# Feed-forward of a routed mixture kernel: second matrix two pieces behind the first, values parted at odd steps, search passes on new steps

## What is computed

```python
scores = scale * np.matmul(q, k.transpose(0, 1, 3, 2)) - np.log(S)
x = np.matmul(1.0 / (1.0 + np.exp(-scores)), v)        # tokens x 768
order = np.argsort(-(x @ w_gate).flatten())            # 8 experts, 224 tokens each
# walk down order: a token goes to the first expert that still has room
h = np.maximum(x[mask] @ w1[e], 0.0)                   # 768 -> 1024
x[mask] = h @ w2[e]                                    # 1024 -> 768
h = x @ w_in                                           # 768 -> 2048
g = np.maximum(h, 0.0) + alpha * np.minimum(h, 0.0)
out = g @ w_out                                        # 2048 -> 768
```

## Time and profile before

| | |
|---|---|
| median of 3 runs | 1059.88 us (1057.77 to 1060.93) |
| the profiled execution | 1057.56 us |
| its span, first to last instruction | 1055.9 us |
| TensorE busy (matmuls) | 971.5 us, 92% |
| VectorE busy | 568.7 us, 54% |
| ScalarE busy | 393.4 us, 37% |
| POOL busy | 187.3 us, 18% |
| mean granted clock | 0.97 of full |

### The profile page before, as it was taken

How to read it: one execution, slowest core, us unless ns; L and a number is a source line. 1 busy time by engine, 2 the same in 40 slices (tenths; PEclk the granted TensorE clock), 3 DMA queues, 4 the chain that set the end, 5 groups by cost and what they waited for, 6 DMA issues and landing times.

```text
span 1055.9 us, 16340 instructions
## 1 busy us (share of the span) xinstructions
PE 971.5 (92%) x6340; PEld 837.9 (79%) x6340; DVE 568.7 (54%) x1289; ACT 393.4 (37%) x629; POOL 187.3 (18%) x202
## 2 busy tenths in 40 slices
PE   4999999806979999899999999999999999999994
PEld 3555555406969898799989998998999999999993
DVE  3344443597566827956953685596448546211110
ACT  3767766501042223355322214542121355222212
POOL 0010011105160010244301014350101326000001
PEclk9999999956989999999999999999999999999998
DMA  9899998407289685956877855579695446966501
GB/s 199 222 265 269 270 265 250 156 17 254 72 236 371 205 225 179 296 133 211 291 283 234 245 169 131 199 233 347 233 243 190 151 123 197 380 231 214 179 1 52
DMA packets 121474, 222.30 MB, mean 211 GB/s; under 512 B 51424, under 2 KB 69216, under 8 KB 121408
## 3 DMA queue, kind: packets, MB, share of 16 engines
q1 hardware_dynamic: 88064, 120.34, 36.7%
q0 software_dynamic: 21280, 91.59, 28.1%
q10 hardware_dynamic: 12064, 9.47, 3.6%
HBM read 184.84 MB, written 36.52 MB: 210 GB/s over the span
## 4 chain that ended last, share of the span: by engine, by line
PE 84%; DVE 9%; ACT 3%; issue 1%; DMA 1%; POOL 1%; ACTq 0%; POOLq 0%; DVEq 0%
PE psum L907 19%; PE psum L895 19%; PE psum L842 11%; PE psum L872 11%; PE psum L644 8%; PE psum L628 7%; DVE hits L1406 4%; PE psum L837 2%; PE psum L612 2%; PE psum L867 2%; PE psum L655 1%; DMA stage<-x_rows,tok_idx 1%; DVE unit L1306 1%; PE psum L789 1%; PE psum L663 1%
## 5 line engine op out<-in xcount | busy, mean ns | idle before, releaser
L907 PE MATMUL psum<-g_high,unit 128*128 128x448 f32 x768 | 231.1, 369 | 4.3 <-DVE g_low L1334 4.1
L895 PE MATMUL psum<-y_high,unit 128*128 128x448 f32 x768 | 230.8, 368 | 4.4 <-ACT below L1041 4.3
L907 PEld LDWEIGHTS psum<-g_high,unit 128*128 128x128 f32 x768 | 144.3, 188 | 18.9 <-DVE g_low L1334 7.7
L895 PEld LDWEIGHTS psum<-y_high,unit 128*128 128x128 f32 x768 | 144.3, 188 | 17.8 <-ACT below L1041 5.8
L907 PE MATMUL psum<-g_low,unit 128*128 128x448 f32 x384 | 140.3, 365 | 0.0
L895 PE MATMUL psum<-y_low,unit 128*128 128x448 f32 x384 | 140.2, 365 | 0.0
L1306 DVE TENSOR_TENSOR unit<-raw,unit 128x768 fp32r<-128x768 f32 (+1 forms) x106 | 109.3, 1060 | 40.3 <-ACT unit L1014 34.9
L1040 ACT ACTIVATE above<-psum 128x448 f32<-128x448 f32 x64 | 34.9, 545 | 248.6 <-PE psum L895 248.6
L1329 DVE SCALAR_TENSOR_TENSOR below<-below,neg_alpha,above 128x448 f32<-128x448 f32 x64 | 43.8, 684 | 146.7 <-ACT below L1041 146.6
L842 PE MATMUL psum<-x_high,unit 128*128 128x224 f32 x672 | 119.4, 279 | 3.0 <-DVE unit L1306 3.0
L872 PE MATMUL psum<-h_high,unit 128*128 128x224 f32 x672 | 115.7, 276 | 1.4 <-issue 1.4
(11 more groups left out here) (168 smaller groups left out, 1260.2 us busy)
## 6 DMA issues: line engine op xcount, KB each, us to landing
unit<-ffn_parts SPq DMA_DIRECT2D x120, 768.0 KB, 5.7
ffn_parts<-pre_parts POOLq DMA_DIRECT2D x24, 768.0 KB, 6.2
ffn_parts<-unit SPq DMA_DIRECT2D x8, 768.0 KB, 5.4
q_in<-in_q_dram SPq DMA_DIRECT2D x24, 224.0 KB, 4.4
k_in<-in_k_dram SPq DMA_DIRECT2D x24, 224.0 KB, 6.1
v_in<-in_v_dram SPq DMA_DIRECT2D x24, 224.0 KB, 6.8
x_rows<-x_tok POOLq DMA_DIRECT2D x8, 672.0 KB, 5.5
rank_in<-suit_flat POOLq DMA_DIRECT2D x6, 896.0 KB
```

What stands on the lines that cost most here:

```text
L895: last = pe.matmul(psum[:, IN_BANK, 0:PAIR], w, y[:, c, :], start=(c == 0 and i == 0), stop=(c == DC - 1 and i == 2))
L907: last = pe.matmul(psum[:, OUT_BANK + d, 0:PAIR], w, g[:, m % 2, :], start=(m == 0 and i == 0), stop=(m == FC - 1 and i == 2))
```

## The change

The order of the feed-forward becomes in 0, in 1, in 2, out 0, in 3, out 1, ..., in 15, out 13, out 14, out 15. Pieces 1 and 2 of w_in add up in banks 6 and 5, the last two of the result, and `ffn_out` of piece 0 waits ahead of column block 4 until they are read. ScalarE waits for g to be parted before `take_in` overwrites its buffers (from m = 2), and for the w_out piece two before ahead of `round_g`. `round_g` and `split_g` move to three steps behind their w_in piece (from m = 2 and from m = 2; piece 1 stays two behind). With it the numbers of the late pieces' steps, the thresholds, flags, indices and selection turns of some rounds move.

```diff
         def in_unit(q, m):
-            return STEPS * q + 2 * OWN + max(2 * m - 1, 0)
+            return STEPS * q + 2 * OWN + max(2 * m - 2, m)
         def out_unit(q, m):
-            return STEPS * q + 2 * OWN + min(2 * m + 2, 2 * FC - 1)
+            return STEPS * q + 2 * OWN + min(2 * m + 3, FC + m)
+        def in_bank(m):
+            return (IN_BANK, OUT_BANK + DC - 1, OUT_BANK + DC - 2)[m] if m < 3 else IN_BANK
...
                 if r == 2:
-                    passes, later = (21, 22, 23, 29, 30, 31, 32, 33), (34, 35, 37, 41)
+                    passes, later = (21, 22, 23, 29, 30, 31, 32, 33), (35, 36, 38, 42)
                 elif r == 3:
-                    passes, later = range(45, 53), (54, 55, 57, STEPS + 5)
+                    passes, later = range(45, 53), (54, 55, 57, STEPS + 7)
                 elif r % 2 == 0:
                     passes, later = (9, 11, 13, 16, 22, 24, 28, 29), (31, 32, 34, 38)
                 else:
-                    passes, later = range(42, 50), (51, 52, 54, STEPS + 3)
+                    passes, later = range(42, 50), (52, 53, 55, STEPS + 5)
...
             def ffn_in(q, m):
-                if m > 0:
+                if m > 2:
                     pe.wait_ge(in_taken, FC * q + m)
...
-                        last = pe.matmul(psum[:, IN_BANK, 0:PAIR], w, y[:, c, :],
+                        last = pe.matmul(psum[:, in_bank(m), 0:PAIR], w, y[:, c, :],
...
             def ffn_out(q, m):
                 for d in range(DC):
+                    if m == 0 and d == DC - 2:
+                        pe.wait_ge(in_taken, FC * q + 3)
...
                 for m in range(FC):
                     ffn_in(q, m)
-                    if m > 0:
-                        ffn_out(q, m - 1)
+                    if m > 1:
+                        ffn_out(q, m - 2)
+                ffn_out(q, FC - 2)
                 ffn_out(q, FC - 1)
...
             def take_in(q, m):
                 act.wait_ge(unit_used, in_unit(q, m) + 1)
+                if m > 1:
+                    act.wait_ge(g_split, FC * q + m - 1)
...
             def round_g(q, m):
                 act.wait_ge(g_made, FC * q + m + 1)
+                if m > 1:
+                    act.wait_ge(unit_used, out_unit(q, m - 2) + 1)
...
-                    if s == in_unit(q, m) + (2 if m > 0 else 1):
+                    if s == in_unit(q, m) + min(m + 1, 3):
                         round_g(q, m)
...
-                        if s0 == in_unit(q, m) + 2:
+                        if s0 == in_unit(q, m) + (2 if m < 2 else 3):
                             split_g(q, m)
```

More of the change, by code:

```diff
@@ L373, in in_unit @@
         def in_unit(q, m):
-            return STEPS * q + 2 * OWN + max(2 * m - 1, 0)
+            return STEPS * q + 2 * OWN + max(2 * m - 2, m)
         def out_unit(q, m):
-            return STEPS * q + 2 * OWN + min(2 * m + 2, 2 * FC - 1)
+            return STEPS * q + 2 * OWN + min(2 * m + 3, FC + m)
+        def in_bank(m):
+            return (IN_BANK, OUT_BANK + DC - 1, OUT_BANK + DC - 2)[m] if m < 3 else IN_BANK
         def ffn_piece(u):
             k = u % STEPS - 2 * OWN
-            return 0 if k == 0 else 2 * FC - 1 if k == 2 * FC - 1 else 2 * ((k + 1) // 2) if k % 2 == 1 else k - 1
+            if k < 2:
+                return 2 * k
+            if k >= 2 * FC - 2:
+                return 2 * (k - FC) + 1
+            return k + 2 if k % 2 == 0 else k - 2
         def width(u):
@@ L1039, in take_in @@
                 act.wait_ge(unit_used, in_unit(q, m) + 1)
-                act.activation(above[:, m % 2, :], psum[:, IN_BANK, 0:PAIR], ACT.Relu)
-                act.activation(below[:, m % 2, :], psum[:, IN_BANK, 0:PAIR], ACT.Relu, scale=-1.0).then_inc(in_taken, 1)
+                if m > 1:
+                    act.wait_ge(g_split, FC * q + m - 1)
+                act.activation(above[:, m % 2, :], psum[:, in_bank(m), 0:PAIR], ACT.Relu)
+                act.activation(below[:, m % 2, :], psum[:, in_bank(m), 0:PAIR], ACT.Relu, scale=-1.0).then_inc(in_taken, 1)
             def round_g(q, m):
                 act.wait_ge(g_made, FC * q + m + 1)
+                if m > 1:
+                    act.wait_ge(unit_used, out_unit(q, m - 2) + 1)
                 act.copy(g_high[:, m % 2, :], below[:, m % 2, :]).then_inc(g_rounded, 1)
```

## The result

The changed kernel takes 1063.03 us (median of 20 runs, 1059.84 to 1069.91) against 1058.70 us for the kernel before (20 runs beside it, 1056.66 to 1062.58): a ratio of 1.0041, 95% interval 1.0026 to 1.0055, so about 4.3 us slower. The forecast was 1055.3 us, in a range up to 1060.0, and faster. Both the sign and the range were wrong.

What follows compares the result with a forecast made beforehand. TensorE's order of work was taken as the bound. Duo 0 -3.1, duo 1 +0.1, duo 2 -0.1, duo 3 -1.4: -4.5 us from 1057.56 gives 1053.1, plus 2.3 for the median 1055.3 us; range 1051.5 to 1060.

Steps and rivals of the forecast that it cites:

- What bounds the kernel: Feed-forward: TensorE's own order of work bounds it, busy 123.6 of 129.8 us in duo 0; reordering gains only its idle time.
- part 1: Feed-forward, all duos: pieces two apart and two more banks remove waits at w_in and w_out pieces, 8.5 us in all.
- Part 2: Feed-forward, duos 0 to 2: values parted at odd steps add a 1.25 us flags wait in each, 3.75 us.
- Part 3: Duo 0's second search: VectorE bounds it; thresholds come 2.5 us earlier, one 3.1 us wait replaces three, duo 0 ends 3.1 earlier.
- rival A: The clock falls behind new waits of 3.1 us in duo 0 and 2.5 in duo 1: 1058.8 us, no change; chance 0.13.
- Part 4, the turns: Outside the feed-forward: selection turns two steps later lose 1.25 us in duo 1 (wait 2.2 to 2.6), 1.0 in duo 2.
- Part 4, last sentence: GpSimd (POOL) queue: w2 gathers behind round 5's and 7's later index still have some 5 us of slack before ScalarE.
- Rival C: w2 gathers of duos 2 and 3 land too late and stop ScalarE's queue: at 9 us lateness 1063.3 us; chance 0.08.

Runs made afterwards that it cites:

- both_even: both_back with the thresholds of rounds 2, 4 and 6 one step later, at even steps: 1056.18 us, ratio 0.9977 to the kernel before.
- search_early: both_even with the eight passes of duo 0's second search (round 3) one step earlier: 1055.72 us, ratio 0.9965 to the kernel before.
- weights_first: The changed kernel with the remaining w2 gathers ahead of the suitabilities' store and spread: 1062.03 us, ratio 1.0038 to the kernel before.
- before_index_late: The kernel before with only round 3's index one step later (58 for 57): 1064.58 us, ratio 1.0059.
- both_back: The changed kernel with selection turns at their old steps and w2 gathers ahead of the suitabilities' store and spread: 1057.58 us, 0.9986 to the kernel before.
- after_again: The changed kernel run again without edit for a second profile: 1065.92 us over 6 runs, ratio 1.0081 to the kernel before; profiled execution 1062.18 us.
- before_turns_late: The kernel before with only the selection turns of the odd rounds two steps later, feed-forward order unchanged: 1062.99 us, ratio 1.0040.
- before_search_early: The kernel before with only the eight passes of round 3 one step earlier, at steps 44 to 51: 1058.70 us, ratio 1.0002.

## Why the prediction was wrong, step by step

**What bounds the kernel, and part 1: right, with one size open.** The waits went: three w_in pieces in a row without a wait, none before w_out's first and last pieces, and F3 -1.4 as foreseen. In F1, with the flags out of the way, the 2.36 measured 2.6 in both_even and only 1.1 in search_early, with the same instructions in F1; the difference is the slower pieces below.

**Part 2: right.** A flags wait of 0.96 to 1.03 us (1.2 to 1.3 with the restart) in each of duos 0, 1 and 2, against 1.25; and it goes when the thresholds stand on even steps.

**Part 3: mechanism right, size off.** One wait replaces three, 2.55 us against 3.1. The threshold matmul starts 439.21 - 337.05 = 102.2 us into the duo, where the earlier trace rows has the thresholds at 440.27 - 336.00 = 104.3; so they come 2.1 us or a little more earlier, against 2.5. But F0 gains 2.0 to 2.15, not 3.1. The rest is the clock: 0.51 from 440.0 to 443.5, right behind that wait. This was rival A's mechanism and nearly its size (a loss of 2.5 less 1.4 hidden); I gave it a chance of 0.13, and it should have been part of the sum. The trace of before had it. The prediction says that no single gap of 3 us stands there, and that reading was wrong: the idle time around 300 in the earlier trace rows ends with one of 3.04. And the clock had fallen before that gap: it stood at 1.00 from 294.70 to 295.80, behind a wait of 2.72 us, and at 0.50 from 295.90 on, where the next wait, of 1.41, had begun (TensorE's timeline, then busy time by stretch):

```profile
294.67 0.80 PE L737 MATMUL psum<-ident,stage 112*128 112x112 f32 x6 [2.72 <-DMA stage<-x_rows,tok_idx]
...
301.30 0.52 PE L842 MATMUL psum<-x_high,unit 128*128 128x224 f32 x1 [3.04 <-DVE unit L1306]
```

```profile
295.90:298.30 2.40, 1.38 (x6) 1.04 (x6) 0.18 (x1) 0.75 (x2) 1.79 (x3) 0.50 0.98 326
```

**Part 4, the turns: place and wait right, price too small.** 2.41 us against 2.2 to 2.6, and H2 +1.0 as worked out. But in H1 the later turns alone cost 4.1 us, not 1.25, since the clock falls behind them as well; rival A had that too. The two falls of the clock that rival A named are worth 1 and some 2.9 us, and with them the forecast would have been about 1059.

**Part 4, last sentence: this is the step that failed.** "Round 5's and 7's index comes one step later, and the six w2 gathers queued behind it on POOL still have some 5 us until ScalarE wants them." I looked at the two rounds whose index step is moved and not at round 3, whose step number stays but whose index comes late all the same: the gather of its rows starts 458.53 - 337.05 = 121.5 us into duo 0 against 456.70 - 336.00 = 120.7 before, and the feed-forward ends 2.1 us earlier: it stands 2.9 us nearer to the expert stretch. That this term is nothing in duo 1 stood in the prediction without a row; the slack there was already nothing (the cast's wait of 0.68 us in the kernel before). The runs showed 3.5 to 5.9 us of wait of TensorE in its place and a further fall of the clock. Rival C had the mechanism, in duos 2 and 3 and with a chance of 0.08; it came in duo 1, where F0's gain and the gathers' loss meet. Shown by weights_first (the wait goes), by before_index_late (the index late in the old order: +6.5 in H1), and by both_back (with both put back, no loss).

For rounds 5 and 7, of which the sentence speaks, its count and its slack are wrong and its price is right. With their index a step later one w2 gather goes ahead of the gather of rows and seven stand behind it, not six (before: none and eight). And ScalarE had no slack there either. Its first cast behind the spread in duo 2, in the kernel before and in the kernel after:

```profile
661.68 0.83 ACT L1014 CAST unit<-raw 128x768 fp32r<-128x768 f32 x1 [1.95 <-DMA raw<-in_moe_w_dram,w_idx]
```

```profile
677.93 0.84 ACT L1025 CAST unit<-raw 128x768 fp32r<-128x768 f32 x1 [3.76 <-DMA raw<-in_moe_w_dram,w_idx]
```

The cast comes 2.7 us into the stretch before and 7.9 after, and TensorE loses nothing by it: H2 is +1.0 as with the late turns alone, H3 0. In duo 1 it is the fourth piece and not one of the first, cast 18.8 us into the stretch; the rounding of the hidden values, which begins 17.4 us into it in the kernel before, has to wait for it. So what counts is how far the late cast stands ahead of the work queued behind it.

Of H1's +9.35 us in after_again, the waits are 3.49 + 2.41 - 1.21 = 4.7 (the last is the wait of the earlier trace rows, gone). That leaves 4.7 for the half clock, which stands there for 3.4 us from 486.2 on and for 6.8 from 499.8 on, 0.6 of them within the second wait: half of the other 9.6 is 4.8. So the clock took about as much as the waits did.

**A term that no rival had: F2.** It should have gained 2.36 - 1.25 = 1.1 us and gained 0.2 to 0.5. Its waits are as foreseen, but the pieces themselves are slower. The chain of waits shows it; start, length and 18 matmuls of one of them, in both_even in duo 2:

```profile
789.90 3.72 PE psum L903 x18
```

The earlier trace rows had 3.65 for the same 18 matmuls, and the granted clock reads 1.00 at both. Among the whole pieces that the chain lists in F2, none takes 3.71 to 3.73 us in the six profiles with the old order, and 11 to 14 do in each of the seven with the new order. Some 12 pieces by 0.07 us are 0.85 us: about what is missing. In F1 it is mixed: none in five profiles of the old order, but 12 in before_turns_late (its +0.8 us there); none in three profiles of the new order and 12 to 14 in four. What makes a piece slower at the same granted clock was not tried, and stays open.

**What follows for the version.** With the two queue edits undone, even threshold steps and the earlier search (search_early), the new order is 0.35% faster than the kernel before (0.21 to 0.50); how much of that is the earlier search the totals leave open. Its largest remaining waits are the flags' in duo 0 (1.29) and those at the w2 matmuls (1.49 in duo 1, 1.87 in duo 2).

## What to carry to other kernels

When a change takes waits out of one stretch, work out for everything queued across its end (here the gathers on GpSimd) how far ahead of its reader it stands, in every stretch and not only in those whose step numbers change: a reader that already waits 0.68 us has no slack, whatever the DMA share says. Price a new wait of TensorE of 2 us or more with the half clock that comes with it, which here cost from 1 us (with a wait of 2.55) to 2.9 (with one of 2.41). And judge an order of work together with the search or load that it exposes: neither the bank alone nor the earlier search alone moved the time, while with the new order, even steps and the two queue edits the ratio was 0.9965.

## What the runs showed of the hardware

- The granted clock fell to 0.50 late in, or within 1 us behind, single waits of 2.41 us (before_turns_late, after), 2.55 us (after), 1.99 us (before_index_late) and 1.82 and 1.87 us (both_back, search_early in H2), in stretches where TensorE was otherwise busy; behind the waits of 1.07 us in the feed-forward, 1.21 in the earlier trace rows, 1.52 in before_search_early and 1.65 in both_back it stayed at 1.00. The page "TensorE: Matmul & The Clock Gate" of the Trainium skill (section "Why this matters for your kernels") warns of idle gaps between bursts, of about the size of the 3.1 us that the prediction worked out. The traces agree that such gaps lower the clock, and differ in the size: here waits of 1.82 us and more did.
- The cast at 483.55 waited for the gather issued at 470.69, the first behind a spread of 896 KB issued at 469.75. From such a gather to the cast that waited for it were 12.9 us there, 12.7 in the kernel before, 12.1 in after_again, 12.3 in before_index_late and, for a w1 piece, 12.5 and 12.7 in weights_first and both_back. That the spread ahead of it makes it so long is argued, not tried.
- The same indirect gather of rows (round 3's) took GpSimd 1.06 us in the kernel before and 3.86 in the kernel after (2.73 in before_index_late); round 5's took 2.74 in the kernel before. Why wasn't tried.
- A piece of 18 matmuls of 448 columns takes 3.65 or 3.72 us at a granted clock of 1.00. Within one kernel it can differ from one execution to the next: all of F3 in the first profile of after is at 3.72 and in the second at 3.65, which is 2.3 us. One piece in the chain of waits of the first, then of the second:

```profile
942.52 3.72 PE psum L917 x18
```

```profile
944.05 3.65 PE psum L917 x18
```
